# Row-sum reciprocals stored to DRAM element by element instead of through TensorE, in an attention and MLP kernel on one Trainium2 core

## What is computed

```python
scores = scale * np.matmul(q_rot, k_rot.transpose(0, 1, 3, 2))
scores = scores - np.max(scores, axis=-1, keepdims=True)
attn = np.exp(scores)
attn = attn / (np.sum(attn, axis=-1, keepdims=True) + 1e-09)
x = np.matmul(attn, v)            # then transposed to 2304 tokens x 512
h = x @ w_in                      # 512 x 2048
g = h * np.tanh(softplus(h))
y = g @ w_out                     # 2048 x 512
```

## Time and profile before

| | before |
|---|---|
| median of 3 runs | 639.32 us (638.94 to 641.34) |
| the profiled execution's own time | 640.83 us |
| its span | 639.0 us |
| PE busy | 617.6 us (97%) |
| DVE, ACT, POOL busy | 338.9, 429.9, 260.1 us |
| packets of the DMA queue q1 | 38576, 59.20 MB, 30.9% of 16 engines |

### The profile page before, as it was taken

The page is one execution under the profiler, slowest core; times in us unless marked ns, Lnnn a source line. Parts: engine busy times, 40 slices in busy tenths (PEclk is TensorE's granted clock), DMA queues, the critical chain, the costliest instruction groups (busy, mean ns, idle before and its releaser), DMA issues.

```text
span 639.0 us, 12703 instructions
## 1 busy us (share of the span) xinstructions
PE 617.6 (97%) x4562; PEld 476.0 (74%) x4562; DVE 338.9 (53%) x577; ACT 429.9 (67%) x691; POOL 260.1 (41%) x208
## 2 busy tenths in 40 slices
PE   3899999999998999999999999999999999999997
PEld 1566666666665669978888888888888888888886
DVE  3677778687786764864433435433534335244331
ACT  2778777787775765666866658675488575586663
POOL 3876878777697258995000530001520006000000
PEclk9999999999999999999999999999999999999999
DMA  6666676567676345040000051000330000000001
GB/s 200 186 202 217 207 228 192 173 205 214 218 219 190 101 135 148 4 129 33 1 0 1 0 136 64 0 1 0 103 94 0 0 0 0 33 33 0 0 0 67
DMA packets 38608, 59.63 MB, mean 93 GB/s; under 512 B 4240, under 2 KB 23824, under 8 KB 38576
## 3 DMA queue, kind: packets, MB, share of 16 engines
q1 hardware_dynamic: 38576, 59.20, 30.9%
HBM read 42.60 MB, written 9.51 MB: 82 GB/s over the span
## 4 chain that ended last, share of the span: by engine, by line
PE 90%; POOL 4%; DMA 2%; DVE 1%; issue 1%; SPq 1%; ACT 0%; DVEq 0%; ACTq 0%; POOLq 0%
PE ps_s L616 14%; PE ps_s L664 13%; PE ps_y L756 10%; PE ps_y L758 10%; PE ps_y L757 10%; PE ps_h L732 9%; PE ps_h L734 9%; PE ps_h L733 9%; PE ps_t L643 7%; DMA xb_l<-reciprocals 1%; POOL wout_lo L556 1%; POOL xb_l L550 1%; PE ps_t L653 1%; POOL xb_h L548 1%; DMA rope_t<-rope 1%
## 5 line engine op out<-in xcount | busy, mean ns | idle before, releaser
L1025 DVE TENSOR_TENSOR h_sb<-h_sb,m_sb 128x1024 f32<-128x1024 f32 x36 | 55.0, 1529 | 144.1 <-ACT m_sb L885 144.1
L954 DVE TENSOR_SCALAR_CACHE_REDUCE minus_s<-ps_s 128x576 f32<-128x576 f32 x144 | 106.3, 753 | 42.2 <-PE ps_s L616 41.5
L822 ACT ACTIVATE prob<-minus_s,neg_max 128x576 f32<-128x576 f32 x128 | 97.9, 768 | 34.6 <-DVE minus_s L954 34.2
L616 PE MATMUL ps_s<-qk_b,qk_a 64*128 64x288 f32 (+1 forms) x320 | 103.3, 453 | 13.8 <-DMA qk_b<-qk_a 10.9
L756 PE MATMUL ps_y<-wout_hi,gh 128*128 128x512 f32 x288 | 112.1, 389 | 0.3 <-POOL wout_lo L556 0.3
L757 PE MATMUL ps_y<-wout_lo,gh 128*128 128x512 f32 x288 | 112.0, 389 | 0.0
L758 PE MATMUL ps_y<-wout_hi,gl 128*128 128x512 f32 x288 | 112.0, 389 | 0.0
L486 POOL TENSOR_TENSOR raw<-raw,rope_t 128x576 f32<-128x576 f32 x62 | 86.5, 1416 | 50.7 <-DMA raw<-qk_in 50.7
L616 PE MATMUL ps_s<-qk_a,qk_b 64*128 64x288 f32 (+1 forms) x320 | 103.3, 454 | 0.0
L732 PE MATMUL ps_h<-xb_h,win_hi 128*128 128x512 f32 x256 | 99.6, 389 | 0.0
L733 PE MATMUL ps_h<-xb_l,win_hi 128*128 128x512 f32 x256 | 99.6, 389 | 0.0
(11 more groups left out here) (58 smaller groups left out, 1030.9 us busy)
## 6 DMA issues: line engine op xcount, KB each, us to landing
raw<-qk_in SPq DMA_DIRECT2D x32, 576.0 KB, 4.4
v_st<-v_in SPq DMA_DIRECT2D x32, 160.0 KB, 2.8
qk_b<-qk_a SPq DMA_DIRECT2D x32, 144.0 KB, 2.5
x_transposed<-xt SPq DMA_DIRECT2D x64, 72.0 KB, 3.1
y_out<-y_mem SPq DMA_DIRECT2D x18, 256.0 KB, 2.0
win_raw<-w_in SPq DMA_DIRECT2D x16, 256.0 KB, 4.8
wout_raw<-w_out SPq DMA_DIRECT2D x16, 256.0 KB, 4.7
x_raw<-x_transposed SPq DMA_DIRECT2D x4, 1024.0 KB, 5.6
```

What stands on the lines that cost most here:

```text
L616: return nc.tensor.matmul(out, q[rows, e, m, cols], k[rows, e, m, r * SIDE:(r + 1) * SIDE], start=True, stop=True)
L822: nc.scalar.activation(dst, minus_s[:, ring(word)].rearrange("p a k -> p (a k)"), ACT.Exp, bias=neg_max[:, col:col + 1], scale=-1.0, accum ...
L954: nc.vector.tensor_scalar(minus_s[:, ring(word)], ps_s[:, score_buf(word, m), :, 0:SIDE], -1.0, None, ALU.mult, ALU.min, accum_out=neg_max ...
```

## The change

The transposes, their copies to SBUF and the waits for them go. `store_r` reads `rec_all` directly, with the partition (the token) as the outer dimension of both sides and the four pairs of the batch as the inner one; successive elements are 36 bytes apart in SBUF and two rows of 2304 tokens apart in DRAM. Each batch takes ten DMAs instead of four. `rec_all` gets memory that lives through the whole kernel.

```diff
+R_PARTS = 16 * 10
...
-        y_mem = both("y_mem", [P, 9 * P])
-        y_sb = y_mem[:, 0:2 * DM].rearrange("p (t n) -> p t n", t=2)
-        rt_late = y_mem[0:PAIRS - EARLY, :].rearrange("p (c t) -> p c t", t=P)
+        y_sb = both("y_sb", [P, 2, DM])
+        rec_all = both("rec_all", [P, PAIRS, 9])
...
             def store_r(b):
-                early = b < EARLY // PB
-                sp.wait_ge(rt_taken, 3 if early else 6)
-                src = rt_early[PB * b:PB * b + PB] if early else rt_late
-                dst = r_d.rearrange("(c a) t -> c a t", a=2)
+                sp.wait_ge(rec_done, 1 if b < EARLY // PB else 2)
+                src = rec_all[:, PB * b:PB * b + PB, :]
+                dst = r_d.rearrange("(c a) t -> a c t", a=2)
                 for e in range(2):
-                    sp.dma_start(dst[:, e, b * S:b * S + FULL], src[:, 4 * e:4 * e + 4, :].rearrange("c t p -> c (t p)")
-                                 ).then_inc(r_stored, 16)
-                    sp.dma_start(dst[:, e, b * S + FULL:b * S + S], src[:, 8, e * D:e * D + D]).then_inc(r_stored, 16)
+                    for t in range(4):
+                        first = b * S + t * P
+                        sp.dma_start(dst[e, :, first:first + P].rearrange("c q -> q c"), src[:, :, 4 * e + t],
+                                     allow_slow_non_contiguous=True).then_inc(r_stored, 16)
+                    sp.dma_start(dst[e, :, b * S + FULL:b * S + S].rearrange("c q -> q c"),
+                                 src[e * D:e * D + D, :, 8], allow_slow_non_contiguous=True).then_inc(r_stored, 16)
...
-            sp.wait_ge(r_stored, 64)
+            sp.wait_ge(r_stored, R_PARTS)
...
-            sp.wait_ge(r_stored, 64 * (EARLY // PB))
+            sp.wait_ge(r_stored, R_PARTS * (EARLY // PB))
...
-            sp.wait_ge(r_stored, 64 * BATCHES)
+            sp.wait_ge(r_stored, R_PARTS * BATCHES)
...
-            pool.wait_ge(rt_done, 6)
...
-            step(12, 0)
-            step(13, 1)
-            for word in TURN_USERS[-2:]:
-                wait_taken(word, 13)
-            turn_reciprocals(0, range(0, 4), 0, 0)
-            turn_reciprocals(0, range(4, 8), 0, 1)
-            turn_reciprocals(0, range(8, 9), 1, 0)
-            for half in range(3):
-                pe.wait_ge(rt_taken, half + 1)
-            for n in range(14, PAIRS + 1):
+            for n in range(2 * LOOP[1], PAIRS + 1):
                 step(n, n % 2)
-            for word in ("G0b-", "G1b-", "G4b-"):
-                wait_taken(word, PAIRS - 1)
-            turn_reciprocals(1, range(0, 4), 0, 0)
-            turn_reciprocals(1, range(4, 8), 0, 1)
-            turn_reciprocals(1, range(8, 9), 1, 0)
...
-            pe.wait_ge(rt_taken, 6)
...
-            act.wait_ge(rt_done, 6)
...
-            act.wait_ge(r_stored, 64 * BATCHES)
...
-            step(13, 1)
-            take_reciprocals(0)
-            for n in range(14, PAIRS + 1):
+            for n in range(13, PAIRS + 1):
                 step(n, n % 2)
...
-            take_reciprocals(1)
...
-            dve.wait_ge(r_stored, 64 * (EARLY // PB))
```

More of the change, by code:

```diff
@@ L200, in attention_mlp @@
         rec_done = sem("rec_done")
-        rt_done = sem("rt_done")
-        rt_taken = sem("rt_taken")
         r_stored = sem("r_stored")
@@ L284, in attention_mlp @@
         sum_all = sb1("sum_all", [P, PAIRS, 9])
-        rec_all = sb1("rec_all", [P, PAIRS, 9])
-        rt_early = sb1("rt_early", [EARLY, 9, P])
         pt = sb1("pt", [P, 2, NT, S])
@@ L667, in p_times_v @@
                 mm.then_inc(pv_done[e], 1)
[L669 to L675, removed]
             def step(n, m):
@@ L983, in reciprocals @@
                 nc.vector.reciprocal(rec_all[:, pairs], sum_all[:, pairs]).then_inc(rec_done, 1)
[L985 to L990, removed]
             def step(n, m):
```

## The result

The changed kernel takes 706.13 us (median of 6 runs, 697.84 to 707.46) against 639.31 us: 1.1015 times the time before, 95% interval 1.0962 to 1.1069. The sign was forecast, the size was not: 655 us with a range to 684.

What follows compares the result with a forecast made beforehand. PE, busy 97% of the span, was taken as the bound. V arriving 14.4 us late, with the 4.2 us gain counted in, plus 1.5 us of slow clock made 16 us on 639.3: 655 us, range 637 to 684.

Steps and rivals of the forecast that it cites:

- The order of the waits: In the attention, PE stands twice for V behind the stores: 4.7 us for V(1, 14), then about 14 us for V(0, 15).
- c: Time of one 4-byte store packet on a DMA engine: taken as 31 ns, bounded by 9 and 61 ns.
- 222.4 + 3e: Arrival of V(0, 15) in us after three batches of stores, forecast at 249.2 us against 234.85 before.
- e: Time of one batch of element stores, 288 packets on each engine: 8.9 us, with ends of 2.6 and 17.6 us.
- A partial write is a read and a write: Rival: each small store to DRAM costs a read and a write, 92 ns; sum 67 us, 707 us; chance 0.16.
- the slow clock: Lower PE clock after the last pause for V, over what is left of the attention: 1.5 us.
- partial writes have a price of their own: Sign for the changed profile: what a c over 61 ns would show about small stores to DRAM.
- The gain of 4.2 us: Removing the early transposes before step 14: 3.1 us of PE's pause plus 1.1 us of slow clock behind it.
- store_r(3) "goes behind the loads of block 1": Last batch of stores, queued after block 1's loads; only block 2 waits for it, some 25 us later: no cost.
- SP's issues, which were to hide: SP's 20 store issues for batches 1 and 2, 6 to 11 us, hidden behind 17.9 us of packets.

Runs made afterwards that it cites:

- alone: Four element-store DMAs of 512 elements, each waited for before the next, in the MLP of the kernel storing rows of ones; 26.3 us from first to last issue.
- after_aligned: The changed kernel with 448 bytes of padding behind rec_all, so the MLP's buffers start at multiples of 512 bytes again; 703.38 us.
- before_shifted: The kernel before the change with one unused tile of 64 bytes a partition ahead of the MLP's buffers; 645.02 us, ratio 1.0094.

## Why the prediction was wrong

**The order of the waits was right.** PE stands for V(1, 14) and then longer for V(0, 15), behind one batch and two. The first batch took 240.84 - 1.36 - 214.85 = 24.6 us, a c of 86 ns; the next two about 38.4 us (247.8 to the landing at 288.3 less 2.1), a c of 67 ns. In 222.4 + 3e these give 285.4 us for V(0, 15); it came at 288.3. That is no test of the steps, since the 38.4 us are read from the same arrival: the rest of 2.9 us is the start of the first store, 214.85 instead of 212.0. The load of V(1, 14) took 8.7 us instead of 4.4. Small stores follow it now, which the old run did not have in such number; that they are the cause was not tried.

**The term that failed is c, the time of one small packet, and with it e.** I took 31 ns, from the window with the smallest packets, and bounded it with 61 ns, from stores of 1152 bytes. That gave 8.9 us for a batch and 14.4 us for the arrival of V(0, 15); measured were 24.6 us for the first batch, 38.4 for the next two, and 53.4 us at that place. Even c at 61 ns gives only 40 us there. Every row of that bound measured how long an engine is busy with a packet of its own size, and took this for the time to the landing. That fails in two ways. The recorded time for a packet of 4 bytes is not one number: 105 ns in the crowded window of the changed kernel, 8 ns in `alone` (25.6% of 16 engines for 1 us, over 518 packets from 483 to 484 us). And the landing comes later than the packets, by 7 us in `alone`. The tests of distance put the price on elements side by side in DRAM; no row of the kernel before had such stores. What DRAM or the path to it does with them stays open.

**The rival that came closest did so by luck.** "A partial write is a read and a write" gave 707 us with a chance of 0.16, and 706 were measured. Its own 67 us were for V(0, 15), where 53.4 were measured; the slow clock, block 1's reciprocals and the moved buffers, of which it had nothing, made up the rest. It also priced each partial write, and writes 64 or 512 bytes apart, just as partial, cost 7.6 to 8.7 us a batch instead of its 26.5. So c came out above 61 ns, which was to show that partial writes have a price of their own, and they have none when they lie apart. What the Trainium skill says on the page "DMA: Bandwidth & Descriptors", section "Specifications", of transfers below 512 bytes does not explain this alone. By the same page's fixed cost of some 3 cycles a packet, in "Why small descriptors are slow (HBM only)", the batch would be hidden. The stores to SBUF (8.4 us) and 64 bytes apart (8.7 us) agree with it as far as SP's issues of some 6 to 7 us let one see, the stores side by side (27 to 33 us) do not.

**The gain of 4.2 us was there.** With row stores it is 4.3 us in the spans and 2.5 in the medians, once the buffers lie as before, and the wait for w_out ends at 277.60 us instead of 281.97. In the changed kernel's own profile PE asked for V(1, 14) at 228.0 us, 2.1 earlier than before and not 4.2. The slow clock behind the pause was part of the cost: in the kernel with the transposes inside, step 14 has a clock of 1.00.

**Two small terms were set to nothing and were not.** store_r(3) "goes behind the loads of block 1": it did, and the load took 4.5 us longer than before, while the stretch to the end of the wait for w_out grew by 3.7. In the kernel with row stores the same load took 9.7 us, so most of it belongs to the element stores; by which way they slow a load ahead of them was not tried. And I gave the move of `rec_all` no cost, since no instruction of the MLP changed. It cost 5.5 us of the 5.7 that the rest of the MLP took longer, by the profile of after_aligned.

The slow clock was put at 1.5 us and cost 2.4. SP's issues, which were to hide, stretched instead: the 20 issues took 29.8 us, not 6 to 11. Whether that alone delayed V was not tried; the load of V behind them took another 13.1 us to land.

## What to carry to other kernels

A store whose elements lie across partitions and side by side in DRAM costs by how densely the elements lie, not by its bytes: a batch of 18 KB took 27 to 33 us to land by itself (19 to 25 in the changed kernel), and 7 to 9 us with the elements 64 bytes or more apart or in SBUF. Price such a store by the time until its semaphore, on the queue in which the next load stands behind it; a window with few packets and few bytes is not a free queue. And when a buffer moves, look at the mean time of the matmuls that read what lies behind it before judging anything else: here 64 bytes cost 4.3 to 5.5 us in the profiles, as much as the whole pause that the change removed (4.2).

## What the runs showed of the hardware that was not expected

- Where a buffer starts in its partition changes TensorE's pace: float32r matmuls of 128 x 512 last 389 ns with all buffers multiples of 512 bytes from the first, and up to 394 ns with most of them 64 bytes off, at the same granted clock; 222 against 219 in 50 us. Only this one displacement was tried, and which operand it is was not separated. Products of `xb_h` with `win_hi` stayed at 389 ns in before_shifted.
- Small stores side by side in DRAM land long after their packets: a DMA of 512 elements alone took over 8 us to its semaphore, its packets about one.
- What stands around them in the queue is slow too: the 512 KB load of x behind batch 0 landed in 16.1 us, where the same load took 4.7.
- With many such stores in the queue SP's own issues last longer: up to 5.6 us for one, where ten stores 64 bytes apart took 5.6 us in all.
